# MoE attention values with the experts' values stationary, the probabilities streaming and the experts paired in column halves

## The reference, cut to what matters

```python
B, S, D, E, Hd, K = 2, 768, 512, 4, 64, 2
logits = x @ w_gate                      # the two largest of four experts for each token
w = softmax over the two selected logits
for e in range(E):
    q, k, v = x @ wq[e], x @ wk[e], x @ wv[e]
    scores = where(causal, -1e9, scale * q @ k.T)
    a = exp(scores - max);  a /= a.sum(-1) + 1e-9
    ye = a @ v @ wo[e]
    out += (w of the tokens that selected e) * ye
```

## Time and profile before

| | us |
|---|---|
| median of 3 runs | 525.22 (524.12 to 527.09) |
| profiled execution, first to last instruction (its span, the only time shown for it) | 524.3 |
| PE busy in it | 483.3 |
| DVE busy in it | 251.9 |
| MoE attention of batch 0, passes 3 to 16 | 102.8 to 151.4 |
| MoE attention of batch 1, passes 3 to 16 | 238.4 to 295.4 |

### The profile page before, as it was taken

One profiled execution on the slowest core, in us unless ns is written; L12 is line 12 of the kernel. 1 busy time (PEld: TensorE's weight loads), 2 busy tenths in 40 slices (PEclk: granted clock), 3 DMA queues, 4 the chain that ended last, 5 costly groups with the idle time before them and its releaser, 6 DMA issues.

```text
span 524.3 us, 8335 instructions
## 1 busy us (share of the span) xinstructions
PE 483.3 (92%) x3252; PEld 419.0 (80%) x3252; DVE 251.9 (48%) x506; ACT 158.3 (30%) x493; POOL 114.4 (22%) x120
## 2 busy tenths in 40 slices
PE   7738699899999798986999999999999999999997
PEld 2526489789887577984898879988998899889985
DVE  4549948575756796758657364211221122112201
ACT  0534434454512476434445121210220022002200
POOL 7449840000008000007920198000000000000000
PEclk9877779999999799998799999999999999999999
DMA  8896492000039501003410067000300040002001
GB/s 250 230 228 147 139 284 76 0 2 2 1 87 225 155 2 63 0 2 90 121 42 0 1 200 241 1 21 21 140 0 20 20 140 0 20 21 82 0 21 40
DMA packets 18210, 41.11 MB, mean 78 GB/s; under 512 B 6320, under 2 KB 6336, under 8 KB 17792
## 3 DMA queue, kind: packets, MB, share of 16 engines
q1 hardware_dynamic: 13952, 27.53, 18.4%
q0 software_dynamic: 2496, 9.97, 6.8%
q10 hardware_dynamic: 1728, 3.15, 1.6%
HBM read 33.17 MB, written 6.29 MB: 75 GB/s over the span
## 4 chain that ended last, share of the span: by engine, by line
PE 76%; DVE 11%; issue 4%; DMA 3%; POOL 2%; SPq 1%; ACT 1%; POOLq 0%; DVEq 0%; ACTq 0%
PE ps_s L468 35%; PE ps_t L468 20%; PE ps_o L468 9%; PE ps_x L468 6%; DMA QT<-in_qT 3%; PE ps_t L591 2%; PE ps_t L508 2%; DVE nmaxA L914 1%; POOL VB L440 1%; DVE US L1067 1%; DVE KL L955 1%; DMA u_rows<-US 1%; DVE nmaxM L1014 1%; SPq L292 1%; PE ps_x L616 1%
## 5 line engine op out<-in xcount | busy, mean ns | idle before, releaser
L468 PE MATMUL ps_s<-UT_h,ch_h 128*128 128x384 f32 x192 | 65.0, 338 | 0.9 <-DVE UT_l L1078 0.9
L468 PE MATMUL ps_s<-UT_h,ch_l 128*128 128x384 f32 x192 | 64.9, 338 | 0.0
L468 PE MATMUL ps_s<-UT_l,ch_h 128*128 128x384 f32 x192 | 64.9, 338 | 0.0
L1152 DVE SCALAR_TENSOR_TENSOR HID_l<-ps_s,HID_h 128x384 fp32r<-128x384 f32 x48 | 26.8, 558 | 74.9 <-ACT HID_h L896 74.9
L468 PE MATMUL ps_t<-ch_h,HID_h 128*128 128x512 f32 x144 | 57.3, 398 | 0.0
L468 PE MATMUL ps_t<-ch_l,HID_h 128*128 128x512 f32 x144 | 56.8, 395 | 0.0
L468 PE MATMUL ps_t<-ch_h,HID_l 128*128 128x512 f32 x144 | 56.8, 394 | 0.0
L896 ACT ACTIVATE HID_h<-ps_s 128x384 fp32r<-128x384 f32 x48 | 23.6, 493 | 105.0 <-PE ps_s L468 105.0
L1158 DVE TENSOR_TENSOR OS<-ps_t,UR 128x512 f32<-128x512 f32 x12 | 8.3, 692 | 86.3 <-PE ps_t L468 86.3
L468 PEld LDWEIGHTS ps_o<-VE,PTM 128*128 128x128 f32 x336 | 42.1, 198 | 3.2 <-issue 2.2
L468 PE MATMUL ps_o<-VE,PTM 128*128 128x64 f32 x336 | 42.3, 279 | 1.3 <-DVE OX L1037 1.0
(11 more groups left out here) (162 smaller groups left out, 985.9 us busy)
## 6 DMA issues: line engine op xcount, KB each, us to landing
KW<-in_kw SPq DMA_DIRECT2D x8, 720.0 KB, 9.6
VW<-in_vw SPq DMA_DIRECT2D x12, 384.0 KB, 8.6
VB<-in_vb SPq DMA_DIRECT2D x4, 768.0 KB, 9.3
QT<-in_qT SPq DMA_DIRECT2D x16, 192.0 KB, 10.7
raw<-in_ch POOLq DMA_DIRECT2D x8, 384.0 KB, 3.4
u_rows<-US ACTq DMA_DIRECT2D x12, 256.0 KB, 3.3
US<-u_rows SPq DMA_DIRECT2D x4, 768.0 KB, 5.7
raw<-in_ch POOLq DMA_DIRECT2D x6, 512.0 KB, 4.2
```

The lines of the kernel that those rows point to most:

```text
L468: return pe.matmul(out, lhsT, rhs, start=start, stop=stop)
L1152: dve.scalar_tensor_tensor(HID_l[:, m, :], bank[m % 4][:, 0:GS], 0.0, HID_h[:, m, :].bitcast(F32), ALU.max, ALU.subtract).then_inc(g_hl, 1)
```

## The change

The operands of `m_values` change places: `VE` (64 columns of one expert) is stationary, the transposed probabilities (128 queries) stream, and the output lies with the 64 features of an expert on 64 partitions of `ps_o` and the queries on its columns. Even experts write partitions 0 to 63, odd ones 64 to 127, in turns. For t=4 and 5 two units are taken together (`VALUES`), so that both halves have work; `PTM` gets a third buffer for this. The output is so already transposed, and `m_out_transpose` goes; the SP queue, which waited for it (`m_ot`) ahead of loading the next batch's second value blocks, waits for `OT_l` (`m_ol`) instead. The weight of each query must now lie along the columns: `m_weights` (DVE) writes gate weight over row sum out to 64 equal columns per expert (`wide`), `m_spread` transposes that on PE into the free half of `ps_o`, and on ACT copies it to `SPREAD`; `m_normalise` multiplies. `OT_h` and `OT_l` are then made from `OX` in SBUF.

In the diff the first `m_spread`, the two loops of `m_values` and the passes are PE's; the second `m_spread` is ACT's, first in its pass; the rest is DVE's, where `m_weights` stands one pass ahead of `m_normalise`.

```diff
+VALUES = [(u,) if UNITS[u][0] < 4 else (u - 1, u) for u in range(MU) if UNITS[u][0] < 4 or UNITS[u][1][0] % 2]
+NVG = len(VALUES)
+GROUP_OF = [next(g for g, us in enumerate(VALUES) if u in us) for u in range(MU)]
...
-                sp.wait_ge(m_ot, b * TQ)
+                sp.wait_ge(m_ol, b * TQ)
...
+            def m_spread(b, t):
+                pe.wait_ge(m_den, b * (3 * TQ) + (3 * t + 3))
+                if t == 0:
+                    pe.wait_ge(m_v2, b * (TQ - NV) + (TQ - NV))
+                else:
+                    pe.wait_ge(m_o, b * TQ + t)
+                for r in range(EP):
+                    last = pe.transpose(ps_o[:, E * HD + r * P:E * HD + (r + 1) * P],
+                                        wide[:, r * P:(r + 1) * P], ident[:, :])
+                last.then_inc(m_d, 1)
...
+                if u == LAST[t]:
+                    pe.wait_ge(m_ds, b * TQ + (t + 1))
+                blocks = [(e, PTM[v % 3], i * UNITS[v][2]) for v in units for i, e in enumerate(UNITS[v][1])]
+                for pair in range(0, len(blocks), 2):
                     for k in range(t + 1):
-                        last = mm(ps_o[:, e * HD:(e + 1) * HD], PTM[:, u % 2, at_:at_ + P],
-                                  VE[:, k, e * HD:(e + 1) * HD], k == 0, k == t)
+                        for e, p_t, first in blocks[pair:pair + 2]:
+                            half = slice(e % 2 * HD, (e % 2 + 1) * HD)
+                            last = mm(ps_o[half, e // 2 * P:(e // 2 + 1) * P], VE[:, k, e * HD:(e + 1) * HD],
+                                      p_t[:, first + k * P:first + (k + 1) * P], k == 0, k == t)
...
                 for k in range(MU + 3):
+                    if k - 3 in LAST:
+                        m_spread(b, LAST.index(k - 3))
                     if k < MU:
                         m_scores(b, k)
...
-                    if k >= 3:
-                        m_values(b, k - 3)
-                    if k in TURN_AT:
-                        m_out_transpose(b, TURN_AT.index(k))
+                    if k >= 3 and k - 3 == VALUES[GROUP_OF[k - 3]][-1]:
+                        m_values(b, GROUP_OF[k - 3])
...
+            def m_spread(b, t): 
+                act.wait_ge(m_d, b * TQ + (t + 1))
+                act.activation(SPREAD[:, t % 2, :], ps_o[:, E * HD:2 * E * HD], ACT.Copy).then_inc(m_ds, 1)
...
+            def m_weights(b, t): 
                 dve.tensor_scalar(denM[:, t % 2, 0, :], sumM[:, t, :], 1e-9, None, ALU.add).then_inc(m_den, 1)
                 dve.reciprocal(denM[:, t % 2, 1, :], denM[:, t % 2, 0, :]).then_inc(m_den, 1)
-                dve.tensor_tensor(denM[:, t % 2, 0, :], denM[:, t % 2, 1, :], gate_w[:, t, :], ALU.mult).then_inc(m_den, 1)
+                dve.tensor_tensor(wide[:, :].rearrange("p (e d) -> p e d", e=E),
+                                  denM[:, t % 2, 1, :].unsqueeze(2).broadcast_to([P, E, HD]),
+                                  gate_w[:, t, :].unsqueeze(2).broadcast_to([P, E, HD]), ALU.mult).then_inc(m_den, 1)
+            def m_normalise(b, t):
+                dve.wait_ge(m_ds, b * TQ + (t + 1))
+                dve.wait_ge(m_av, b * NVG + (GROUP_OF[LAST[t]] + 1))
+                dve.tensor_tensor(OX[:, t % 2, :], ps_o[:, 0:E * HD], SPREAD[:, t % 2, :], ALU.mult).then_inc(m_o, 1)
             def m_out_lo(b, t):
-                dve.tensor_tensor(OT_l[:, :, :], ps_x[:, 0:EP * P].rearrange("p (k s) -> p k s", k=EP),
+                dve.tensor_tensor(OT_l[:, :, :], OX[:, t % 2, :].rearrange("p (k s) -> p k s", k=EP),
                                   OT_h[:, :, :].bitcast(F32), ALU.subtract).then_inc(m_ol, 1)
```

More of the change, by code:

```diff
@@ L122, in program @@
         denM = sb("denM", [P, 2, 2, E], F32)
+        gate_at = place[0]
         gate_max = sb("gate_max", [P, TQ], F32)
@@ L128, in program @@
         gate_rank = sb("gate_rank", [P, TQ, E], F32)
+        wide, end_wide = at("wide", [P, E * HD], F32, gate_at)
+        assert end_wide <= place[0]
         gate_w = sb("gate_w", [P, TQ, E], F32)
         gate_s = sb("gate_s", [P, 2, TQ], F32)
+        us1_at = place[0]
         US1 = sb("US1", [P, NUS, DM], F32)
@@ L163, in program @@
         PM, p = at("PM", [P, 3, 1024], F32, p)
-        PTM, p = at("PTM", [P, 2, 1024], F32, p)
+        PTM = [None, None, None]
+        for i in range(2):
+            PTM[i], p = at(f"PTM{i}", [P, 1024], F32, p)
+        PTM[2], spread_at = at("PTM2", [P, 1024], F32, us1_at)
+        SPREAD, end_spread = at("SPREAD", [P, 2, E * HD], F32, spread_at)
+        assert end_spread <= region1
         region5 = max(p, endA)
@@ L240, in program @@
         m_den = sem("m_den")
+        m_d = sem("m_d"); m_ds = sem("m_ds")
         m_o = sem("m_o")
-        m_ot = sem("m_ot"); m_oh = sem("m_oh"); m_ol = sem("m_ol")
+        m_oh = sem("m_oh"); m_ol = sem("m_ol")
         m_wo = sem("m_wo")
@@ L318, in _ @@
                     load_queries(b, r)
[L319 removed]
+                sp.wait_ge(m_av, b * NVG)
                 load_blocks(b, 0)
@@ L593, in m_transpose, with m_values @@
                 last.then_inc(m_t, 1)
-            def m_values(b, u):
-                t, experts, stride = UNITS[u]
+            def m_spread(b, t):
[8 more added lines that the diff above has]
+                last.then_inc(m_d, 1)
+            def m_values(b, g):
+                units = VALUES[g]
+                t, u = UNITS[units[0]][0], units[-1]
                 pe.wait_ge(m_pt0, b * MU + (u + 1))
@@ L599, in m_values @@
                     pe.wait_ge(m_pt1, b * BANK1[MU] + BANK1[u + 1])
-                if u == 0:
+                if units[0] == 0:
                     pe.wait_ge(m_v2, b * (TQ - NV) + (TQ - NV))
-                if experts[0] == 0 and t >= 1:
+                if UNITS[units[0]][1][0] == 0 and t >= 1:
                     pe.wait_ge(m_o, b * TQ + t)
-                for i, e in enumerate(experts):
+                if u == LAST[t]:
+                    pe.wait_ge(m_ds, b * TQ + (t + 1))
+                blocks = [(e, PTM[v % 3], i * UNITS[v][2]) for v in units for i, e in enumerate(UNITS[v][1])]
+                for pair in range(0, len(blocks), 2):
                     for k in range(t + 1):
-                        at_ = i * stride + k * P
-                        last = mm(ps_o[:, e * HD:(e + 1) * HD], PTM[:, u % 2, at_:at_ + P],
-                                  VE[:, k, e * HD:(e + 1) * HD], k == 0, k == t)
+                        for e, p_t, first in blocks[pair:pair + 2]:
+                            half = slice(e % 2 * HD, (e % 2 + 1) * HD)
+                            last = mm(ps_o[half, e // 2 * P:(e // 2 + 1) * P], VE[:, k, e * HD:(e + 1) * HD],
+                                      p_t[:, first + k * P:first + (k + 1) * P], k == 0, k == t)
                 last.then_inc(m_av, 1)
[L611 to L617, removed]
             def m_out_project(b, t):
@@ L622, in m_out_project @@
                 pe.wait_ge(m_ol, b * TQ + (t + 1))
+                if t >= 1:
+                    pe.wait_ge(m_xl, b * TQ + t)
                 split3(ps_x[:, :], range(EP), lambda k: OT_h[:, k, :], lambda k: OT_l[:, k, :],
@@ L819, in m_to_sbuf @@
                 act.wait_ge(m_t, b * MU + (u + 1))
-                if u >= 2:
-                    act.wait_ge(m_av, b * MU + (u - 1))
-                act.activation(PTM[:, u % 2, 512:512 + width], ps_t[:, 1, 0:width], ACT.Copy).then_inc(m_pt1, 1)
+                if u >= 3:
+                    act.wait_ge(m_av, b * NVG + (GROUP_OF[u - 3] + 1))
+                act.activation(PTM[u % 3][:, 512:512 + width], ps_t[:, 1, 0:width], ACT.Copy).then_inc(m_pt1, 1)
+            def m_spread(b, t):
+                act.wait_ge(m_d, b * TQ + (t + 1))
+                if t == 0:
+                    act.wait_ge(st_u[2], b * (16 * TQ // NUS) + 16)
+                act.activation(SPREAD[:, t % 2, :], ps_o[:, E * HD:2 * E * HD], ACT.Copy).then_inc(m_ds, 1)
             def m_out_hi(b, t):
-                act.wait_ge(m_ot, b * TQ + (t + 1))
-                act.activation(OT_h[:, :, :], ps_x[:, 0:EP * P].rearrange("p (k s) -> p k s", k=EP),
+                act.wait_ge(m_o, b * TQ + (t + 1))
+                if t >= 1:
+                    act.wait_ge(m_wo, b * TQ + t)
+                act.activation(OT_h[:, :, :], OX[:, t % 2, :].rearrange("p (k s) -> p k s", k=EP),
                                ACT.Copy).then_inc(m_oh, 1)
@@ L1022, in m_to_sbuf @@
                 dve.wait_ge(m_t, b * MU + (u + 1))
[L1023 to L1027, removed]
+                if u >= 3:
+                    dve.wait_ge(m_av, b * NVG + (GROUP_OF[u - 3] + 1))
+                if u == 2:
+                    for i in range(2):
+                        dve.wait_ge(st_u[i], b * (16 * TQ // NUS) + 16)
+                dve.tensor_copy(PTM[u % 3][:, 0:width], ps_t[:, 0, 0:width]).then_inc(m_pt0, 1)
+            def m_weights(b, t):
                 dve.tensor_scalar(denM[:, t % 2, 0, :], sumM[:, t, :], 1e-9, None, ALU.add).then_inc(m_den, 1)
```

(2 more changed lines are left out.)

10 lines of the change are left out of this document (2 added, 8 removed).

## The result

The changed kernel takes 532.7 us (median of 4 runs, 530.92 to 533.59), the kernel before beside it 526.15 (4 runs, 524.12 to 528.48): ratio 1.0139, 95% interval 1.0088 to 1.0189. The forecast was 525.1, range 520 to 530.5. The profiled execution spans 531.8 us (its time 533.58).

A forecast was written before the change was run, and what follows sets the result against it. PE was taken as the limit (483.3 of 524.3 us busy), DVE in passes 3 and 4. Batch 0 +1.4 and batch 1 -1.5 gave 524.2; the median stands 0.9 above: 525.1, range 520 to 530.5.

The forecast's parts named there:

- passes 3 and 4, batch 0: First spread holds queued PE work until the gates and `wide` finish, +3.3 us; clock falling behind that wait, +2.0.
- pass 5 on, batch 0: 72 cheaper value blocks -6.0 us, an earlier PE wait gone -0.5, new waits +2.6: sum -3.9.
- passes 3 and 4, batch 1: PE waits over 8 us for `wide` beside POOL, then half clock; end at 256.1 against 252.97: +3.1 us (2.6 to 4.3).
- pass 5 on, batch 1: -3.9 us as in batch 0, -1.4 for the earlier slow clock, +0.9 for POOL, -0.2 for last out-transposes: -4.6.
- The wait for `wide`: Passes 3 and 4, batch 0: PE's first spread waits 4.3 us for gates and weights, the second 1.1.
- the row of 2.88 us: Earlier profile's PE wait of 2.88 us, followed by 6.4 us at clock 0.50; basis for predicting the clock's fall.
- The waits of passes 12 to 16: Batch 0, new PE waits: spread in pass 12, 0.6 us; transposes in pass 14, 1.15; spread, copy and values in pass 16, 0.85.
- slower by POOL: Rival: `OT_l` and `wide` wait for POOL five times in passes 4 to 8 of batch 1, +3: 528.1 us, chance 0.08.
- slower by the clock: Rival: clock stays at half until pass 5 in both batches, +2.0, +1.2 and +0.9: 529.2 us, chance 0.14.
- The price of a block: Value matmuls: 0.135 us per block for 0.218 before, bounds 0.107 and 0.215, saving 7.0 us per batch.

The follow-up runs named there:

- e7: The changed kernel run again without any edit, beside other follow-up kernels: 532.25 us, ratio 1.011 to the kernel before.
- e5: Changed kernel plus idle matmuls ahead of the first spread's wait, 16 in batch 0 and 40 in batch 1: 526.43 us, ratio 1.001 to before.
- e2: Changed kernel with the spread moved behind scores and transposes, still ahead of the values, which wait for ACT's copy: 529.31 us, ratio 1.009 to before.
- e6: Changed kernel, spread behind the values without their wait for its copy, POOL's weight splitting held until batch 1's second value group: 512.79 us, ratio 0.976.
- e9: Changed kernel, 16 idle matmuls ahead of each batch's first spread wait, POOL's weight splitting held until batch 1's second value group: 522.69 us, ratio 0.995.
- e3: Changed kernel with POOL's weight splitting held until batch 1's second group of values is done: 524.53 us, ratio 1.001 to before.

## Why the prediction was wrong, step by step

| term | predicted | measured | |
|---|---|---|---|
| passes 3 and 4, batch 0 | +3.3 + 2.0 = +5.3 | +5.0 | right |
| pass 5 on, batch 0 | -3.9 | -2.9 | gain a quarter less |
| **passes 3 and 4, batch 1** | **+3.1** | **+7.8** | **the term that failed** |
| pass 5 on, batch 1 | -4.6 | -3.3 | gain a quarter less |

Measured is A and B, changed less before. The rest of the span's 7.5 us, -1.84 between the batches and +2.6 ahead of them, is in the profiled executions; e7 had 1.5 less between and 0.65 more ahead.

**Right.** The wait for `wide` was 4.07 (said 4.3), the second 1.37 (1.1), and the clock went to half until 112.6 (said 112 or 113), at a price of 1.3 to 1.4 us by e5 (said 2.0):

```profile
109.70:112.60 2.90, 2.82 (x12) 2.21 (x13) 0.47 (x2) 0.38 (x1) 0.00 (x0) 0.50 0.00 0
```

That it would fall during the wait was in part luck. In the row of 2.88 us it was taken from, the 1.62 us behind the wait (175.98 to 177.60) still had 0.95, and e2 shows it fall behind a wait of 1.71 us, where the prediction had one of 1.6 leave it at 1.00.

The waits of passes 12 to 16 came about as listed (0.6, 1.15, and 0.85 for the last spread and ACT's copy):

```profile
141.44 0.44 PE L608 MATMUL ps_o<-ident,wide 128*128 128x128 f32 x2 [0.44 <-DVE wide L1062]
...
147.23 0.84 PE L596 MATMUL ps_t<-ident,PM 128*128 128x128 f32 x6 [1.03 <-DVE PTM L1053]
148.37 0.50 PE L473 MATMUL ps_x<-wo_h,OT_h 128*128 128x512 f32 x1 [0.30 <-DVE OT_l L1073]
...
154.83 1.53 PE L473 MATMUL ps_o<-PTM,VE 128*64 128x128 f32 x24 [0.56 <-ACT SPREAD L843]
```

**The step that failed** is the one on batch 1: "So `wide` ends at 246.7", "`m_weights` of t=1 waits for POOL until 251.8", "end at 256.1 if the clock is back by 253.5". Three sizes were off, one behind the other:
- From the end of the gates to the end of `wide` I gave 1.6 us (246.7 - 245.07). It took 3.4 (247.97 to 251.35): `denM` was held up until the cast ended, and `wide` then met the subtraction, 1.88. I had let POOL hold DVE up once, for one cast: +1.75.
- From the first spread to the second I gave 5.9, with the clock at half in it; it took 7.57. The weights of t=1 could start after 4.7, 0.4 sooner than I had said. But they took 2.4 for the 0.8 given, as `wide` was again 1.88, and the spread also waits for `OX` of t=0 behind them, 0.4, which I had left out: +1.7.
- From the second spread to pass 5 I gave 3.5; it took 4.72, with a mean granted clock of 0.64. I had the clock back by then; it had come back, for the spread and the first scores lasted as at full clock (0.41, 0.48), and it fell to half a second time: +1.2. The stretch from the second spread to pass 5:

```profile
258.98:263.70 4.72, 4.72 (x30) 3.35 (x31) 1.92 (x2) 1.57 (x5) 4.25 (x6) 0.64 0.39 105
```

The sum, 4.65, is the term's error of 4.7. The rivals had both parts, but apart: *slower by POOL* in passes 4 to 8 with 0.08, *slower by the clock* with 0.14. They do not exclude each other. They act in the same 12 us and feed each other: POOL makes the wait longer, the clock falls behind it, slow scores hold DVE up, and DVE meets POOL again. As rivals with a price each they gave 529.2 and 528.1. The two prices added to 525.1 would have come to 532.2; that this meets the measured time is chance, since the first has 2.0 in batch 0, where the clock did as summed, and the gain of B was 2.3 too large.

**The price of a block** was 0.122 to 0.129 in groups of 8 blocks and more, where I took 0.135. But about 0.1 us goes by ahead of each group, from the transposes or the projection to the first value (121.80 to 122.11, 0.31 for 0.23 elsewhere in the six projection matmuls); with that the 72 blocks took 9.1 + 0.8 us, as the 9.7 predicted. So the value matmuls' work was right, and the missing 1.0 in batch 0 is small change around them: those 0.2; the wait of 0.28 for OT_l, which I had let go with the 0.5 of before and which stayed (0.30); and the last spread and what it waits for, 1.3 us (from 153.53, the end of the matmul of 153.30 with its 0.23, to 154.83), where I gave 0.85. In batch 1 there is POOL besides: OT_l took 1.03 at 264.68 and `wide` 1.71 at 267.76, for 0.42, and the spread of t=2 waited 1.24 for it.

**What the place of the spread costs** in passes 2 to 4, from e6, e9, e5 and e7. Both batches have 9.76 with the spread behind the values. Ahead of the scores it is 12.91 even with full clock and idle POOL: 3.15 each. This is what is left when both are taken away; I put it down to PE and DVE waiting for each other, as their rows in the changed kernel show, and no run takes it apart further. The clock adds 1.4 in batch 0 (14.34 - 12.91) and 4.7 in batch 1 (23.66 - 18.98), POOL 6.1 in batch 1 (18.98 - 12.91). That is 18.5 us, of which the kernel before had 6.0 itself (15.78 in batch 1 against e6's 9.76). Each A is read from one profiled execution. How clock and POOL share in batch 1 depends on which is taken first: with POOL late the clock is worth 1.3 there (14.24 - 12.91).

## What to carry to other kernels

A small product for the end of a chain (here the gate weights) should not stand ahead of independent work on an engine that runs in order: 0.4 us of transposes held back 6 us of scores and values. The same transposes behind the values, with nothing but `m_normalise` left to wait for their copy, turned +1.1% into -1.6%; ahead of the values they still cost 0.9%. Where a new wait is found, price it together with what is slow beside it; two penalties that each look unlikely can come together and lengthen each other. And stationary values in column halves pay mainly in turns: 0.125 us per block of 128 queries by 128 keys in turns, 0.195 one half after the other, 0.218 in the old form.

## What had not been expected of the hardware

The same wait in the same code is followed by clocks of different length. In e3, batch 0 is the code of the changed kernel, and its first spread waited the same 4.07 us (row 107.70); behind it

```profile
108.04:118.48 10.44, 9.54 (x55) 6.84 (x53) 4.48 (x8) 3.41 (x9) 0.00 (x0) 0.56 0.01 2
```

took 10.44 us at a mean of 0.56, for 8.42 at 0.84 in e7 and 7.14 at 1.00 in e5. So the clock's price behind one such wait was 1.3 us or 3.3, from one execution to another, which puts the same spread on what the clock costs in the table. Why is open. And idle matmuls, 3.6 us of work in batch 0 and 8.8 in batch 1 that nobody reads, made the kernel 5.8 us faster.
